# Block means three steps earlier, fused weight groups two val groups later: attention, gated convolution and spatial MLP on one core

## The reference, cut to what matters

```
k_sum = k.reshape(B, H, nb, block, D).max(axis=3)
v_sum = v.reshape(B, H, nb, block, D).mean(axis=3)
scores = concat(where(|i - j| < 16, scale * q @ k.T, -1e9), scale * q @ k_sum.T + log(block))
x = softmax(scores) @ concat(v, v_sum)              # heads side by side: (2, 768, 512)
gate = sigmoid(sum_k conv_w[k] * x shifted by k)
y = (gate * (x @ w_val)) @ w_out
h = relu(y @ w_in); u, v = halves of h
v_n = (v - mean) / sqrt(var + 1e-6)
out = (u * (w_spatial @ v_n + b_spatial)) @ w_out2
```

## Time and profile before

| what | value |
|---|---|
| median of 3 runs | 308.56 us (308.08 to 308.92) |
| profiled execution, its own time | 308.57 us |
| its span | 306.8 us |
| PE busy | 293.8 us, 96% of the span |
| DVE busy | 173.9 us, 57% |
| ACT busy | 150.9 us, 49% |
| POOL busy | 123.4 us, 40% |
| DMA | 25.52 MB, mean 83 GB/s |

### The profile page before, as it was taken

One profiled execution on the slowest core, in us unless ns is written; L12 is line 12 of the kernel. 1 busy time (PEld: TensorE's weight loads), 2 busy tenths in 40 slices (PEclk: granted clock), 3 DMA queues, 4 the chain that ended last, 5 costly groups with the idle time before them and its releaser, 6 DMA issues.

```text
span 306.8 us, 5354 instructions
## 1 busy us (share of the span) xinstructions
PE 293.8 (96%) x1768; PEld 268.6 (88%) x1768; DVE 173.9 (57%) x578; ACT 150.9 (49%) x464; POOL 123.4 (40%) x140
## 2 busy tenths in 40 slices
PE   7789999999999999989999999999999999999996
PEld 6788888988889899887999998888899999988885
DVE  5899888998788867778300006787755242310000
ACT  3689999999997764442422234433332111122221
POOL 6434887777534884223300001343476323220000
DMA  7999999984610633000000001121010000002222
GB/s 160 213 207 233 228 194 185 252 225 117 168 49 0 189 88 103 0 2 0 1 2 0 0 2 51 51 80 41 35 34 2 0 0 2 0 35 90 83 103 103
DMA packets 51801, 25.52 MB, mean 83 GB/s; under 512 B 44586, under 2 KB 46910, under 8 KB 51774
## 3 DMA queue, kind: packets, MB, share of 16 engines
q1 hardware_dynamic: 51774, 25.18, 33.6%
HBM read 22.03 MB, written 3.15 MB: 82 GB/s over the span
## 4 chain that ended last, share of the span: by engine, by line
PE 63%; ACT 20%; issue 7%; DVE 6%; POOL 2%; DMA 1%; ACTq 0%; DVEq 0%; POOLq 0%
PE psum L697 54%; ACT probs L833 7%; DVE psum L1050 4%; ACT probsT L847 2%; ACT qT L821 2%; PE psum L654 2%; ACT xT L856 2%; ACT psum L875 2%; PE psum L673 1%; PE psum L613 1%; PE psum L578 1%; ACT xT L853 1%; PE psum L785 1%; PE psum L627 1%; DVE gate L1050 1%
## 5 line engine op out<-in xcount | busy, mean ns | idle before, releaser
L526 POOL TENSOR_TENSOR g_lo<-work,g_hi 128x384 fp32r<-128x384 f32 x32 | 32.3, 1024 | 46.9 <-ACT g_hi L957 26.2
L526 POOL TENSOR_TENSOR vn_lo<-work,vn_hi 128x512 fp32r<-128x512 f32 x12 | 15.5, 1293 | 61.3 <-DVE vn_hi L1152 61.3
L833 ACT ACTIVATE probs<-neg_s,neg_max 128x120 f32<-128x120 f32 x96 | 37.0, 392 | 0.7 <-DVE neg_max L976 0.5
L642 PE MATMUL psum<-probsT,v_win 120*128 120x128 f32 x192 | 29.9, 278 | 0.0
L613 PE MATMUL psum<-k_win,qT 128*128 128x120 f32 x192 | 29.0, 274 | 0.8 <-DVE qT L1014 0.7
L976 DVE CUSTOM_DVE_ANT_0 neg_s<-psum,mask 128x120 f32<-128x120 f32 x96 | 24.6, 277 | 5.2 <-PE psum L613 4.8
L1050 DVE SCALAR_TENSOR_TENSOR psum<-xT,conv_c,psum 128x384 f32<-128x384 f32 x48 | 26.0, 616 | 1.2 <-ACT psum L875 1.0
L613 PEld LDWEIGHTS psum<-k_win,qT 128*128 128x128 f32 x192 | 25.2, 191 | 1.2 <-issue 0.9
L642 PEld LDWEIGHTS psum<-probsT,v_win 120*128 120x128 f32 x192 | 25.2, 191 | 0.8 <-issue 0.2
L1130 DVE TENSOR_TENSOR wsp_lo<-psum,wsp_hi 128x384 fp32r<-128x384 f32 x12 | 6.6, 549 | 33.3 <-ACT wsp_hi L938 33.3
L957 ACT ACTIVATE g_hi<-work 128x384 fp32r<-128x384 f32 x16 | 8.3, 523 | 34.6 <-DVE work L1164 34.6
(11 more groups left out here) (125 smaller groups left out, 721.1 us busy)
## 6 DMA issues: line engine op xcount, KB each, us to landing
v_win<-in_v_dram SPq DMA_DIRECT2D x16, 240.0 KB, 3.3
k_nat<-in_k_dram SPq DMA_DIRECT2D x16, 192.0 KB, 5.0
v_nat<-in_v_dram SPq DMA_DIRECT2D x8, 384.0 KB, 3.9
out_dram<-work SPq DMA_DIRECT2D x11, 256.0 KB, 2.0
q_nat<-in_q_dram SPq DMA_DIRECT2D x14, 192.0 KB, 4.4
raw<-in_moe_w_spatial_dram SPq DMA_DIRECT2D x6, 384.0 KB, 3.1
raw<-in_moe_w_out_dram SPq DMA_DIRECT2D x8, 256.0 KB, 2.8
raw<-in_moe_w_in_dram SPq DMA_DIRECT2D x8, 256.0 KB, 2.8
```

The source lines that it names most:

```text
L526: nc.gpsimd.tensor_tensor(dst_lo, src, dst_hi.bitcast(F32), ALU.subtract).then_inc(lo_sem, 1)
L642: ins = nc.tensor.matmul(bank_x(i)[:, i % 2 * 2 + g, :], v_win[0:KEYS, s, 2 * t + g, :], probsT[0:KEYS, i % 2, g, :], start=True, stop=True)
L833: ins = nc.scalar.activation(probs[:, i % RING, g, :], neg_s[:, i % 3, g, :], ACT.Exp, bias=neg_max[:, i % 4, g:g + 1], scale=-1.0, accum_ ...
```

## The change

The means of pairs 2 to 7 go from step 6p + 2 to step 6p - 1, the last step of the pair in front; those of pairs 0 and 1 stay. SyncE loads `v_nat` of pair 1 ahead of the loop and that of pair p + 2 inside it, and POOL runs `add_v` a pair ahead. The first four fused groups stand behind val groups 7, 9, 11 and 13 in place of 5, 7, 9 and 11, and VectorE does the convolution of the next channel block before it takes such a group.

```
+        means_at = [2, T + 2] + [T * p - 1 for p in range(2, PAIRS)]
...
             load_v(0)
+            load_v_nat(1)
             for p in range(PAIRS):
                 if p + 2 < PAIRS:
                     load_heads(p + 2, k_h, k_nat, k_loaded, k_turned)
                 if p >= 1:
                     load_v(p)
-                if p + 1 < PAIRS:
-                    load_v_nat(p + 1)
                 if p + 2 < PAIRS:
+                    load_v_nat(p + 2)
                     load_heads(p + 2, q_h, q_nat, q_loaded, q_turned)
...
+            add_v(0)
             for p in range(PAIRS):
-                add_v(p)
+                if 2 <= p < PAIRS - 1:
+                    add_v(p + 1)
                 if p >= 2:
                     split_x(p - 2)
                 spread_means(p)
+                if p == 1:
+                    add_v(2)
                 if p + 1 < PAIRS:
                     k_tails(p + 1)
+                if p == 0:
+                    add_v(1)
...
-                if (i + 2) % T == 0 and i + 2 < STEPS:
-                    pe.wait_ge(v_mean_ready, (i + 2) // T + 1)
+                if i == 0 or i + 4 in means_at:
+                    pe.wait_ge(v_mean_ready, 1 if i == 0 else means_at.index(i + 4) + 1)
...
-                if p < PAIRS and t == 2:
-                    means(p)
+                if i in means_at:
+                    means(means_at.index(i))
...
-                if p < PAIRS and t == 2:
-                    take_means(p)
+                if i in means_at:
+                    take_means(means_at.index(i))
...
                 if kind == "fused":
+                    if n < len(FUSED_AFTER):
+                        while taps < min(LATER * (FUSED_AFTER[n] // 2 + 3), LATER * B * C):
+                            conv(taps)
+                            taps += 1
                     dve.wait_ge(fused_hi_ready, n + 1)
...
-FUSED_AFTER = (5, 7, 9, 11)
+FUSED_AFTER = (7, 9, 11, 13)
```

## The result

| | before | after |
|---|---|---|
| median of the runs beside each other | 308.62 us (308.08 to 308.92, 4 runs) | 304.28 us (303.87 to 305.81, 4 runs) |
| profiled execution, own time | 308.57 us | 304.14 us |
| its span | 306.8 us | 302.4 us |

The kernel became faster, with a ratio of 0.987 and a 95% interval of 0.9833 to 0.9907. The forecast was 306.6 us with a range from 305.0 to 308.2 us. A small spread comes from the clock: an execution whose mean granted TensorE clock was 0.994 instead of 1.00 took longer, both here (305.81 us against 303.87 to 304.43 for the other three) and for the half hoist further down (304.78 and 305.74 us against 303.17 and 303.69).

A forecast was written before the change was run, and what follows sets the result against it. ScalarE was taken to bound the attention and TensorE the convolution and the dense tail. 308.57 - 2.35 + 0.96 (means) + 1.2 (load) - 1.8 (fused groups) = 306.6 us, range 305.0 to 308.2 us for 8 in 10.

The forecast's parts named there:

- The bound: TensorE has no gap from 135.8 to 304 us; the change can only move that start forward or back.
- The fused groups, 1.8 less: Convolution: TensorE's loss of 2.62 us goes, but for 0.8 us of waiting at the third fused group.
- Rival 3: Convolution: the wait only moves to the third fused group; 308.4 us, no change; chance 0.13.
- The load, 1.2 more: First pairs: v_nat put ahead of k of pair 2 makes k land 1.2 us later, and nothing absorbs it.
- rival 4: The load costs only its issue, 0.64 us, and the new step hides nearly all the means; 304.9 us; chance 0.16.
- POOL and the scores, nothing: Near step 11: POOL's earlier add_v of pair 2 (1.00 us) still leaves TensorE's scores on time, costing nothing.
- The means, 2.35 less and 0.96 more: Attention: five old ScalarE waits of 0.47 us go; six new ones of 0.16 us come; net 1.39 us less.
- Pair 7: Attention, about 80 us: the copy behind this pair's means had no such wait, so nothing goes there.
- Rivals 1 and 2: Attention: means not hidden, 311.2 us, chance 0.07; or VectorE or loads hold pairs at 10 us, 308.0, chance 0.12.

The follow-up runs named there:

- half hoist: Changed kernel with only four of the eight convolution instructions in front of the taking of a fused group: 304.23 us, ratio 0.9849.
- k first: Changed kernel with v_nat of pair 1 loaded behind k of pair 2 again: 303.23 us, ratio 0.9813.
- a third of the matmuls at the new place: Changed kernel with one of the three matmuls of each means, output not the reference's: 303.82 us, ratio 0.9832.
- The kernels with one edit each: Kernel before with only VectorE's convolution ahead of the taking of fused groups, 306.81 us; or with only the later fused-group places, 308.28 us.
- the kernel with the loads alone: Kernel before with v_nat loads and add_v a pair ahead, means and fused groups as before: 309.7 us, ratio 1.0033.
- the means part alone: Changed kernel without the two edits of the fused part, so means moved, loads and add_v a pair ahead: 306.29 us, ratio 0.9925.

## Why the prediction was right and wrong

- **The bound.** Right: the dense tail kept its length, and all of the gain lies ahead of it.
- **The fused groups, 1.8 less.** Right in size (1.80) and mechanism: one wait at the third fused group, 0.54 us plus what TensorE loses in starting again, 0.82 us lost against the 0.8 computed. That the sizes agree to 0.02 is partly luck, since the same wait is 0.87 us in two other traces (k first, and a third of the matmuls at the new place). The kernels with one edit each add that the hoist does it nearly alone. Rival 3 didn't occur.
- **The load, 1.2 more.** Right in kind, and somewhat too big: 0.89 in the trace, 0.87 in the mean over all traces, about 1 us as the ratio of the kernel with the loads alone. The k load landed 1.0 us later, not 1.2. Of that, 0.47 us are the issue of `v_nat` ahead of it (12.68 to 13.15 in SP's queue), some 0.1 a queue that was late already (12.68 for the place that k had at 12.56), and 0.3 a longer way from issue to landing (4.2 against 3.9). In the six traces with `v_nat` ahead, this way takes 4.2 to 4.8 us (mean 4.45), in the five with the old order 3.8 to 4.3 (mean 3.96). So issue and landing have about equal parts, and the value lies between the 0.64 of rival 4 and the 1.2 taken. The order of the landings in the changed kernel (the `v_nat` issued at 12.7 at 16.2, the second half of k at 17.9) agrees with what I cited from the Trainium skill on ring order in one queue (DMA: Bandwidth & Descriptors, Queues, rings and completion order). But that section of the Trainium skill gives the order in which descriptors are taken, says that a later one may finish its write before an earlier one, and has no price. So my "cannot overtake" went beyond it, and it was no ground for taking 1.2 rather than 0.64.
- **POOL and the scores, nothing.** Right.
- **The means, 2.35 less and 0.96 more. This is the step that failed**, in its sizes: the net term was -1.39 and measured -3.37. Four things make up the difference of 1.98.
  - *The old wait was bigger than the 0.47 shown.* The idle time is counted from the end of the instruction that reads the accumulator behind the exponential. But where nothing is waited for, ScalarE's next instruction starts before that end. The distance of the copies shows the true stall: 1.61 to 1.04, 0.57 us. Five times 0.10 is 0.5 us.
  - *The new wait is hardly there.* I took 1.18 us from the means' start to the copy, measured where TensorE had waited before. Behind running work it is 1.08, and ScalarE arrived almost then. The last step became only 0.04 to 0.05 us longer, not 0.16: about 0.7 us for six pairs.
  - *ScalarE's own copy is not just moved.* It costs 0.46 in its new place and freed 0.58 in the old one. I had put nothing down here; it is some 0.7 us for six pairs.
  - *Pair 7* gained 0.10 where I had said that nothing goes. Against it stand 0.15 us lost once in pair 2's last step (1.75 instead of 1.60); the trace of the means part alone doesn't have them, and it has 3.52 us where this one has 3.37. Together with the other three this gives 1.85 to 1.9 of the 1.98.

The range was too narrow for the same reason: its best case took the sum of the waits shown, 2.35 us, as the most that could be gained by the means, and a sum of shown waits is no such limit. It was also added too narrowly: its own bounds, added up, give 304.8 to 308.3 us and not 305.3 to 307.9, and even that leaves 304.28 out. Rival 4 (0.16) came nearest with 304.9 us. Its picture of the new step, nearly all hidden, is what happened; it too had the old wait at 2.35. Rivals 1 and 2 fell plainly: no wait of ScalarE in the pairs, and a period of 9.30 us with VectorE at 8.99.

## What to carry to other kernels

Take the worth of removing a wait from the distance between two recurring instructions of the bounding engine, compared with a step that has the same work and no wait, not from the idle time shown. In a pipeline of equal rounds, count what stands between two takings of a bank in the rounds of each engine: moving long work ahead of a wait shortened the round here, and half of the move was better than all of it, since the bank came free earlier. A load put ahead of one that an engine already waits for showed up here almost in full (1.0 us later landed, 0.89 us later started), so move such a load only if its own consumer needs it.

## What the runs showed of the hardware

**A shown idle time was 0.1 us too small on ScalarE.** Two stretches of its timeline, kernel before with the wait and after it without:

```profile
49.99 0.38 ACT L833 ACTIVATE probs<-neg_s,neg_max 128x120 f32<-128x120 f32 x1
50.28 0.19 ACT L833 ACTIVATION_READ_ACCUMULATOR probs<-neg_s,neg_max 128x1 f32 x1
50.94 0.38 ACT L847 ACTIVATE probsT<-psum 120x256 f32<-120x256 f32 x1 [0.47 <-PE psum L627]
```

```profile
50.19 0.38 ACT L841 ACTIVATE probs<-neg_s,neg_max 128x120 f32<-128x120 f32 x1
50.47 0.19 ACT L841 ACTIVATION_READ_ACCUMULATOR probs<-neg_s,neg_max 128x1 f32 x1
50.57 0.37 ACT L855 ACTIVATE probsT<-psum 120x256 f32<-120x256 f32 x1
```

Without a wait the copy starts 0.38 us after the exponential, while the read still runs until 50.66. With it, it starts 0.95 us after: 0.57 lost, 0.47 shown.

**The means' matmuls cost less behind running work.** The three matmuls of the means are six in the trace (x6). In the new step the transposes follow the means' start after 0.66 us (0.82 busy), in the old one after 0.76 us (0.92 busy). In the old step there was a gap ahead of them, since the means also had to wait for ScalarE's copy of the step in front; in pair 3 that copy starts at 39.37:

```profile
39.28 0.38 PE L578 MATMUL psum<-ident,k_nat 128*128 128x128 f32 x2
39.81 0.92 PE L654 MATMUL psum<-v_nat,sel 128*120 128x128 f32 x6
40.56 0.38 PE L627 MATMUL psum<-ident,probs 128*120 128x128 f32 x2
```

```profile
39.37 0.38 ACT L847 ACTIVATE probsT<-psum 120x256 f32<-120x256 f32 x1
...
40.98 0.38 ACT L847 ACTIVATE probsT<-psum 120x256 f32<-120x256 f32 x1 [0.47 <-PE psum L627]
```

This is the loop that set the old step: copy to means 0.44, means to transposes 0.75, transposes to copy 0.42, together 1.61 us. ScalarE's own work in it is 1.04. In the new step the means start 0.21 us behind the start of the two transposes ahead of them, where that was 0.53.

**The start of the kernel varies.** The fifth step's copy, which doesn't wait for the load of k of pair 2, started between 16.15 and 17.13 us in the thirteen profiled executions, and the two orders of the loads overlap there (16.15 to 16.74 for the old one, 16.29 to 17.13 with `v_nat` ahead). Part of it vanished in the wait for k one step later, so a difference of two single traces at that place carries some tenths of a microsecond that aren't the edit's.

**Open:** why a step with both the x copies and the copy of the means takes 0.10 to 0.12 us more than the sum. With the copy of the means in that step, the x copy starts only when the accumulator read is over (52.32 + 0.19, then 52.53 before; in the changed kernel 51.50 + 0.19, then 51.59), though no wait is shown. Whether any small copy in that step does this is not shown.
